# Attention with two MLP layers on one core: batch 0's probabilities turned by TensorE, and a new spread of the MLP's half steps

## The reference

```python
# q, k, v: (4 batches, 8 heads, 576, 64)
scores = scale * q @ k.T
thresh = max(scores, -1) - tau
scores = where(scores >= thresh, scores, -1e9)
attn = exp(scores - max); attn = attn / (sum(attn) + 1e-9)
x = (attn @ v) laid out as 2304 tokens x 512
# layer 0: 512 -> 2048 -> 512
h = x @ w_in;  x = (s * relu(h)**2 + b) @ w_out
# layer 1: 512 -> 2048 -> 512
h = x @ w_in2; out = (h * sigmoid(1.702 * h)) @ w_out2
```

## Time and profile before

| what | value |
|---|---|
| time, median of 3 runs | 1167.25 us (1165.93 to 1169.19) |
| profiled execution | 1167.29 us, its span 1165.5 us |
| PE busy | 1043.8 us (90%) |
| DVE, ACT, POOL busy | 652.5, 650.4, 732.7 us |
| PE busy tenths in 40 slices | 3655678988889988988899999999999999999998 |
| granted TensorE clock over the span | 0.969 of full speed |
| chain that ended last | PE 67%, DVE 15%, POOL 6%, DMA 4% |

### The profile page before, as it was taken

One profiled execution on the slowest core, in us unless ns is written; L12 is line 12 of the kernel. 1 busy time (PEld: TensorE's weight loads), 2 busy tenths in 40 slices (PEclk: granted clock), 3 DMA queues, 4 the chain that ended last, 5 costly groups with the idle time before them and its releaser, 6 DMA issues.

```text
span 1165.5 us, 18156 instructions
## 1 busy us (share of the span) xinstructions
PE 1043.8 (90%) x6024; PEld 915.4 (79%) x6024; DVE 652.5 (56%) x1598; ACT 650.4 (56%) x1215; POOL 732.7 (63%) x773
## 2 busy tenths in 40 slices
PE   3655678988889988998899999999999999999998
PEld 2444467867778877877799999999999998989897
DVE  6988998888889888988223223232222222222222
ACT  3344345665666666666467676654545445454543
POOL 4566556766868777776366566656666666666663
PEclk9976789999999999999999999999999999999999
DMA  3566676787787877766543333433434444444442
GB/s 111 135 160 162 143 180 164 166 187 178 174 199 173 191 184 179 194 168 171 134 127 118 120 125 127 127 121 123 151 125 149 129 126 153 127 154 127 154 127 81
DMA packets 119451, 173.23 MB, mean 149 GB/s; under 512 B 30912, under 2 KB 86336, under 8 KB 119360
## 3 DMA queue, kind: packets, MB, share of 16 engines
q1 hardware_dynamic: 119360, 172.08, 54.7%
HBM read 124.85 MB, written 4.72 MB: 111 GB/s over the span
## 4 chain that ended last, share of the span: by engine, by line
PE 67%; DVE 15%; POOL 6%; DMA 4%; SPq 3%; ACT 2%; issue 2%; DVEq 0%; ACTq 0%; POOLq 0%
PE y_ps L356 28%; PE scores L341 25%; PE shared L341 6%; PE scores L307 5%; DVE scores L413 5%; DVE prob L437 4%; DVE blocks L450 3%; PE scores L286 3%; SPq L225 3%; POOL w_lo L679 3%; DMA prob_t<-blocks 3%; POOL prob L672 1%; POOL q_hl L653 1%; DVE limit L420 1%; DMA qk_raw<-qk 1%
## 5 line engine op out<-in xcount | busy, mean ns | idle before, releaser
L679 POOL TENSOR_TENSOR w_lo<-raw_slab,w_hi 128x512 fp32r<-128x512 f32 x384 | 498.1, 1299 | 291.5 <-ACT w_hi L556 291.0
L473 DVE TENSOR_TENSOR g_lo<-gate,g_hi 128x384 fp32r<-128x384 f32 x192 | 117.8, 614 | 223.9 <-ACT g_hi L584 223.9
L556 ACT CAST w_hi<-raw_slab 128x512 fp32r<-128x512 f32 x384 | 236.0, 616 | 6.1 <-DMA raw_slab<-slabs_a 4.2
L356 PE MATMUL y_ps<-w_lo,g_hi 128*128 128x512 f32 x576 | 227.2, 394 | 0.0
L356 PE MATMUL y_ps<-w_hi,g_lo 128*128 128x512 f32 x576 | 226.8, 394 | 0.0
L356 PE MATMUL y_ps<-w_hi,g_hi 128*128 128x512 f32 x576 | 224.6, 390 | 0.0
L535 ACT ACTIVATE prob<-scores,neg_max 128x576 f32<-128x576 f32 (+1 forms) x160 | 118.5, 740 | 184.3 <-DVE scores L413 181.5
L467 DVE TENSOR_TENSOR gate<-scores,gate 128x384 f32<-128x384 f32 x136 | 75.8, 557 | 194.8 <-ACT gate L566 140.3
L341 PE MATMUL scores<-act_hi,w_hi 128*128 128x384 f32 x544 | 184.7, 340 | 0.0
L341 PE MATMUL scores<-act_hi,w_lo 128*128 128x384 f32 x544 | 183.5, 337 | 0.0
L341 PE MATMUL scores<-act_lo,w_hi 128*128 128x384 f32 x544 | 182.6, 336 | 0.0
(11 more groups left out here) (47 smaller groups left out, 1471.5 us busy)
## 6 DMA issues: line engine op xcount, KB each, us to landing
raw_slab<-slabs_a SPq DMA_DIRECT2D x96, 512.0 KB, 4.2
raw_slab<-slabs_b SPq DMA_DIRECT2D x96, 512.0 KB, 3.5
prob_t<-blocks SPq DMA_DIRECT2D x192, 100.0 KB, 4.1
qk_raw<-qk SPq DMA_DIRECT2D x32, 576.0 KB, 5.4
prob_t<-blocks SPq DMA_DIRECT2D x192, 80.0 KB, 3.7
v_sb<-v SPq DMA_DIRECT2D x16, 320.0 KB, 3.2
out<-rows_b SPq DMA_DIRECT2D x18, 256.0 KB, 4.0
prob_t<-blocks SPq DMA_DIRECT2D x64, 60.0 KB, 2.9
```

The costliest lines, as they stand in the source:

```text
L356: mm = nc.tensor.matmul(y_ps[g][:], gp[:, n % 2, toks], wp[n % W_RING][:, w], start=(f == 0 and k == 0), stop=(f == SLABS - 1 and k == 2))
L473: nc.vector.tensor_tensor(g_lo[:, n % 2, :], gate[:, n % 2, :], g_hi[:, n % 2, :].bitcast(F32), ALU.subtract).then_inc(g_lo_ready, 1)
L556: nc.scalar.copy(w_hi[n % W_RING][:, cols], raw_slab[:, n % 2, cols]).then_inc(w_hi_ready, 1)
L679: nc.gpsimd.tensor_tensor(w_lo[n % W_RING][:, cols], raw_slab[:, n % 2, cols], w_hi[n % W_RING][:, cols].bitcast(F32), ALU.subtract).then_ ...
```

## The change

- Batch 0 (heads 0 to 7) is cut into tiles of 128, 128, 128, 128, 64 rows; the other batches as before (rows_of, cut_of). Its q columns are no longer reordered.
- For these 40 tiles TensorE turns the normalised probabilities, three slots behind their scores: four transposes into y_ps[0] or y_ps[1], a fifth (the last 64 keys) into y_ps[2], for a head's fifth tile into "shared". These banks belong to the MLP, which starts later. ACT copies them into prob_t, or, for pairs 0 and 2, into the idle blocks buffers. DVE's turn and the DMA moves are left for batches 1 to 3.
- Batch 0's contexts are three pieces of 192 columns a pair, at slots 10 x pair + 14, + 16, + 18. Contexts of the other batches come at + 17 to + 20; their moves keep their slots.
- Half steps: 32 over the slots 48 to 91 (8 in 11 slots), from slot 92 on six in five slots; 127 are done at slot 170. The first four slabs are split one part a slot in slots 38 to 45.
- ACT's affine and g_hi come in the slot after the hidden product, g_lo on DVE one later; the turned rows' x_hi and x_lo stand ahead of the gate steps.

```diff
-MLP_FROM = 51
-SECOND_FROM = 91
+MLP_FROM = 48
+SECOND_FROM = 92
+PIECES = [(pair, THIRD * n, THIRD, 2 * TPH * pair + 14 + 2 * n)
+          for pair in range(PAIRS_PER_BATCH) for n in range(3)]
+PIECES += [(pair, RUN * a, QUAD_RUNS[a], 2 * TPH * pair + 17 + a)
+           for pair in range(PAIRS_PER_BATCH, PAIRS) for a in range(QUADS)]
 def halves_by(slot):
+    if slot < SECOND_FROM:
+        return max(0, (2 * SLABS * (slot - MLP_FROM + 1)) // (SECOND_FROM - MLP_FROM))
+    full, rest = divmod(slot - SECOND_FROM, 5)
+    return 2 * SLABS + 6 * full + [1, 3, 4, 5, 6][rest]
+            def turn_tile(j):            # TensorE, in slot j + 3, behind the scores
+                h, t = divmod(j, TPH)
+                m = rows_of(j)
+                if j == 0:
+                    pe.wait_ge(ident_loaded, 16)
+                pe.wait_ge(normed, j + 1)
+                if j >= 2:
+                    pe.wait_ge(main_copied, j - 1)
+                for c in range(KEY_CHUNKS - 1):
+                    nc.tensor.transpose(y_ps[j % 2][:, c * m:(c + 1) * m], prob[0:m, j % PROBS, c * P:(c + 1) * P],
+                                        ident[0:m, 0:m])
+                if t < TPH - 1:
+                    if t == 0 and h >= 1:
+                        pe.wait_ge(tail_copied, h)
+                    place = y_ps[2][0:64, t * P:t * P + m]
+                else:
+                    if h >= 1:
+                        pe.wait_ge(last_copied, h)
+                    place = shared[0:64, 0:m]
+                nc.tensor.transpose(place, prob[0:m, j % PROBS, (KEY_CHUNKS - 1) * P:SEQ], ident[0:m, 0:m]
+                                    ).then_inc(rows_pe_turned, 1)
+            def copy_turned(j):          # ACT, in slot j + 3
+                h, t = divmod(j, TPH)
+                m, q0 = rows_of(j), cut_of(j)
+                act_eng.wait_ge(rows_pe_turned, j + 1)
+                if t == 0 and h >= 4:
+                    act_eng.wait_ge(context_ready, pieces_of(h // 2 - 1))
+                nc.scalar.copy(prob_t_of(h)[:, 0:KEY_CHUNKS - 1, q0:q0 + m],
+                               y_ps[j % 2][:, 0:(KEY_CHUNKS - 1) * m].rearrange("p (c q) -> p c q", q=m)
+                               ).then_inc(main_copied, 1)
...
             # DVE
-            for slot in range(SLOTS):
+            for slot in range(SLOTS + 2):
                 if 0 <= slot - 1 < TILES:
                     mask(slot - 1)
+                if slot - 1 in PIECE_OF:
+                    context_lo(slot - 1)
                 for u in halves_of(slot - 1):
-                    mlp(u)
+                    rows_due(u)
+                for n in hidden_in(slot - 1):
+                    gated(n)
+                for n in hidden_in(slot - 2):
+                    gated_lo(n)
...
             # ACT
+            for slot in range(SLOTS + 1):
                 h, t = divmod(slot, TPH)
+                for n in hidden_in(slot - 1):
+                    affine(n)
                 if slot < TILES:
                     exponent(slot)
+                if slot in PIECE_OF:
+                    context_hi(slot)
+                if 0 <= slot - TURN_LAG < PE_TILES:
+                    copy_turned(slot - TURN_LAG)
+                for n in hidden_in(slot - 1):
+                    gated_hi(n)
                 for u in halves_of(slot):
+                    rows_due(u)
+                for n in hidden_in(slot):
+                    gate_of(n)
+                for u in halves_of(slot):
+                    rows_and_weights(u)
```

More of the change, by code:

```diff
@@ L25 @@
 BLOCKS = SEQ // BLK
-ROWS = [128, 128, 128, 96, 96]
-TPH = len(ROWS)
-CUTS = [sum(ROWS[:t]) for t in range(TPH)]
+ROWS_PE = [128, 128, 128, 128, 64]
+ROWS_DVE = [128, 128, 128, 96, 96]
+TPH = len(ROWS_DVE)
 RUN = TPH * BLK
@@ L186, in build, with prob_t_of @@
         out_written = sem("out_written")
+        def prob_t_of(h):
+            if h < PE_HEADS and h // 2 % 2 == 0:
+                return blocks[h % 2][:].rearrange("p b t j -> p (b t j)").rearrange("p (c q) -> p c q", q=SEQ)
+            return prob_t[h % 2]
         pure_from = halves_by(SLOTS - 1)
@@ L505, in _ @@
                     invert(slot - 2)
-                if 0 <= slot - 3 < TILES:
-                    turn(slot - 3)
-            for u in range(halves_by(SLOTS - 2), HALVES):
-                mlp(u)
+                if PE_TILES <= slot - TURN_LAG < TILES:
+                    turn(slot - TURN_LAG)
+            for u in range(pure_from, HALVES):
+                n = u // 2
+                if n < STEPS and 2 * n >= pure_from:
+                    if u % 2 == 0:
+                        gated(n)
+                    else:
+                        gated_lo(n)
+                rows_due(u)
         @block.scalar
@@ L637, in _ @@
                     split_k(h + 1)
-                if slot in W_EARLY:
-                    for part in range(2):
-                        slab_hi(W_EARLY.index(slot), part)
+                if W_EARLY <= slot < W_EARLY + 2 * W_RING:
+                    slab_hi(*divmod(slot - W_EARLY, 2))
             for u in range(pure_from, HALVES):
-                if u % 2 == 1 and u // 2 < STEPS:
-                    affine(u // 2)
-                mlp(u)
+                n = u // 2
+                if n < STEPS and 2 * n >= pure_from:
+                    if u % 2 == 0:
+                        gate_of(n)
+                    else:
+                        affine(n)
+                        gated_hi(n)
+                rows_due(u)
+                rows_and_weights(u)
         @block.gpsimd
@@ L699, in _ @@
                     split_k(h + 1)
-                if slot in W_EARLY:
-                    for part in range(2):
-                        slab_lo(W_EARLY.index(slot), part)
+                if W_EARLY <= slot < W_EARLY + 2 * W_RING:
+                    slab_lo(*divmod(slot - W_EARLY, 2))
                 for u in halves_of(slot):
```

212 lines of the change are left out of this document (116 added, 96 removed).

## The result

| | before | after |
|---|---|---|
| median, us | 1167.5 (11 runs) | 1171.63 (11 runs, 1168.77 to 1175.65) |
| ratio after / before | | 1.0035, 95% interval 1.002 to 1.0049 |
| span of the profiled execution, us | 1165.5 | 1170.2 |
| forecast, us | | 1148 (range 1137 to 1167) |

A forecast was written before the change was run, and what follows sets the result against it. A 2.50 us round of row_max, exp and mask bounds slots 0 to 50, TensorE the end after the slots; -7.1 - 3.4 - 8.9 = -19.4 on the 1165.5 us span, plus 1.8, gives 1148 us, range 1137 to 1167.

The forecast's parts named there:

- A plain slot stays 2.50: Batch 0 slots: a round of row_max, exp, mask sets 2.50 us, so removing 40 DVE transposes gains 0.
- behind scores(slot) and ahead of scores(slot+1): Batch 0's 200 transposes in TensorE's queue: next scores stay over 0.5 us early, cost 0; +20 if cover goes.
- The clock is up when a pair's first context comes: Batch 0: transposes fill TensorE's slots, so first contexts run at full clock; only one cold context, 1.6 us, counted.
- A: Stage from row_max of slot 0 to that of slot 50, 142.1 us before; forecast 135.0, a change of -7.1.
- Rival 1: Clock stays low in batch 0: four first contexts each pay 1.6 us, +4.9 in all, 1153 us; chance 0.15.
- 12 x 0.5: Batch 0's twelve context pieces of 192 columns, each lengthening its slot by 0.5 us over a plain 2.50.
- B, -3.4: Slots 50 to 92, 142.8 us before: -2.4 fewer halves, -5.0 DMA waits, +4.0 ACT wait.
- +4.0: Slots 50 to 92: ACT's g_hi waits for an output two slots on, four times; +5.1, taken as +4.
- C and D, -8.9: From slot 92 to the end: 2.1 later half, -5 DMA waits, -4 idle filled, -2 paired slots and turns.
- 12.4 forecast: From slot 92: TensorE's act_lo wait at paired slots, 4 x 2.5 + 8 x 0.3, against 14.6 before.
- -4: From slot 92: denser halves shrink TensorE's 5.6 + 3.0 us of waiting for DVE; bounds 0 and -8.6.
- 4 x 2.5: From slot 92: four turns where a hidden step directly follows an output, each waiting 2.5 us for act_lo.

The follow-up runs named there:

- turns_behind_context: Changed kernel, but batch 0's transposes and ACT copies that stood just ahead of a context come behind its scores; 1164.22 us, ratio 0.9950 to the kernel before.
- fill_transposes: Changed kernel plus eight transposes of the identity behind scores in slots 0 to 47 with t 0 to 2, no context; 1165.66 us, 0.9980 of the kernel before.
- fill_matmuls: Changed kernel plus four unused 512-column matmuls behind scores in slots 0 to 47 with t 0 to 2, no context; 1159.19 us, 0.9935 of the kernel before.
- schedule_odd_even: schedule_alone, but in slots 51 to 91 each odd half step comes in the slot right behind its even one; 1153.48 us, 0.9872 of the kernel before.
- schedule_alone: Kernel before, batch 0 still on DVE and DMA, with the new half-step spread, contexts at + 17 and later g_hi, g_lo; 1154.96 us, ratio 0.9883.
- schedule_steady: schedule_alone with one half step a slot from slot 92 on instead of six in five; 1161.42 us, ratio 0.9947 to the kernel before.
- before_filled: Kernel before plus four unused 512-column matmuls in slots 0 to 50 with t below 4 and no context; 1166.90 us, ratio 0.9987.

## Why the prediction was wrong, step by step

- **"A plain slot stays 2.50", the transposes buy nothing.** Right: 2.48 to 2.51 in most of batch 0's plain slots.
- **The transposes on TensorE, priced at 0 from "behind scores(slot) and ahead of scores(slot+1)".** This step failed. The bound was set against the next scores alone. In nine slots the next thing in the queue is a context, which with its scores fills the slot by itself. In six of them the rows come in time and the context starts 0.17 to 0.19 us after row_max all the same. In the other three, the first contexts of slots 14, 24 and 34, the rows come 3.0 us into their slot instead of the 2.0 of the earlier trace rows, because a head's k split stands ahead of them on GpSimd; the context starts 1.7 us late, and this goes straight into the round: 5.1 us in all. Taking the transposes away gave 7.6 us (turns_behind_context), 5.1 in the first contexts' slots and 2.8 in those of the contexts 18 and 38, which then ran at the high clock. The 2.0 us of the earlier trace rows were not laid against the context slots, nor against GpSimd's splits.
- **"The clock is up when a pair's first context comes".** Failed. The clock did rise long before the first context, but it was down again when that came. The averages, 0.84 in A against the 0.81 of the earlier trace rows, mislead: in the kernel before the granted clock reads 1.00 from 10 to 50 us, though the scores matmuls there have the durations of the low level (0.79 to 0.85 us, in the changed kernel 0.53 at the high one). From 50 us on it is 0.74 before and 0.83 after, so the transposes did raise it, too little. The timeline of slots 11 and 12 shows the two scores matmuls at 0.53 us, a wait of 1.78 for GpSimd, and then 0.85:

```profile
38.14 0.53 PE L331 MATMUL scores<-k_hi,q_hl 128*128 128x288 f32 x2
...
40.72 0.68 PE L353 MATMUL y_ps<-ident,prob 64*128 64x64 f32 x4 [1.78 <-POOL prob L782]
...
41.44 0.85 PE L331 MATMUL scores<-k_hi,q_hl 128*128 128x288 f32 x2
```

Rival 1 named this and sized it well for the first contexts: it counted four times 1.6 us, and the four took 6.0 us more than at the high clock. But four later contexts (slots 18, 38, 46, 48) were cold too, 3.47, 2.47, 3.37 and 3.12 us instead of 1.85, another 5.0 that stood in no step. A rule by which transposes do not count for the clock is not the reason, as fill_transposes shows. When exactly the clock falls stays open: in fill_matmuls the same wait of 1.6 us stands ahead of the contexts of slots 24 and 34, and one ran at 3.47, the other at 1.85.
- **"12 x 0.5" for contexts.** Mis-sized: standing alone, a context makes its own slot 2.78 and the next one 3.01, so 0.8 rather than 0.5, 3.5 us in all. With the late start and the low clock gone A is 136.2 us, near the forecast 135.0; the new cut and ACT's copies are in it, so they cost little, as forecast.
- **B, -3.4.** Measured -0.1. The DMA waits of TensorE went as forecast, 6.6 us to none in B and 6.6 to 0.3 in C. The step had priced only that side of the later context: DVE's turn now waits for free blocks (2.5 us in B, 10.7 in C, neither of them before), and TensorE's waits for masks ahead of scores grew from 3.9 to 13.0 in B. Which of these ate the 3.4 us was not tested. The wait on ACT came as forecast, 8.1 us in four waits (about 10 said); schedule_odd_even shows that it cost little, so the +4.0 priced for it was too much.
- **C and D, -8.9.** Measured -6.8, in part by luck. The waits from 306 to 596 us of the changed kernel:

```profile
PE shared L416 <- DVE act_lo L559: 13.1, 7, 3.3
...
DVE blocks L530 <- DMA prob_t<-blocks: 10.7, 12, 1.9
...
PE shared L416 <- POOL w_lo L789: 5.0, 6, 1.3
...
ACT w_hi L658 <- DMA raw_slab<-slabs_a: 4.6, 6, 1.2
```

TensorE waits for act_lo 13.1 us against 12.4 forecast. Its waits for masks and context splits, 5.6 + 3.0 before, are gone whole, where -4 was taken, and the waits for w_lo are new. The four paired turns wait 3.15, 3.32, 1.39 and 2.89 us, 10.8 against 4 x 2.5. In the timeline of slot 98 a part of it is DVE's wait for free blocks, which stands ahead of the mask and x_lo; and the hidden product behind drops to the low clock in the middle (0.33 to 0.52 us a matmul):

```profile
330.58 0.78 DVE L530 STREAM_TRANSPOSE blocks<-prob 128x576 f32<-128x576 f32 x1 [1.95 <-DMA prob_t<-blocks]
...
332.22 0.54 DVE L559 TENSOR_TENSOR act_lo<-shared,act_hi 128x384 fp32r<-128x384 f32 x1
...
332.91 0.41 PE L416 MATMUL shared<-act_hi,w_hi 128*128 128x384 f32 x1 [3.15 <-DVE act_lo L559]
333.16 0.33 PE L416 MATMUL shared<-act_lo,w_hi 128*128 128x384 f32 x1
...
334.39 0.52 PE L416 MATMUL shared<-act_lo,w_hi 128*128 128x384 f32 x1
334.71 0.52 PE L416 MATMUL shared<-act_hi,w_lo 128*128 128x384 f32 x1
```

- **The wait of the hidden product for w_lo** stood in no step. It is new, 5.0 us in C (7.8 in schedule_alone, 2.2 in schedule_steady); the weight loads of the same product had waited 4.3 us for it in C before, and wait 10.1 now. The denser halves overtake GpSimd. One of the prediction's own signs of being wrong came with it: casts waited for raw_slab, 4.6 us in six waits, where the kernel before had one of 0.4.

## What to carry to other kernels

When work is put into an in-order queue, price it against every item that can follow it, and by when its own inputs come. Here it was free in front of 0.8 us of scores and in front of six contexts for which the rows came in time, and cost 1.7 us in front of each of three contexts for which GpSimd was late. A matmul burst behind a half idle stretch can pay in clock as well as in waiting: here 11 us in A, of which a few unused matmuls or transposes in the gaps gave most back, and all only once the late start was gone too. When two repairs together give the sum of each alone, look at the slots before calling them separate. Split a change of many parts by stage and time the parts alone, and then check that they add up: here one half alone won 1.2%, the other alone lost 0.4%, and together they lost 0.35%.

## What the runs showed of the hardware

Four matmuls of 512 columns or eight transposes in three slots of five (none where a context stands) raised the granted clock from 50 to 154 us from 0.83 to 0.97, and shortened stage A by 10.0 and 10.3 us, though TensorE had more to do. Three of the four first contexts were still slow in either (2.87, 3.47 and 3.11 us with the matmuls, 2.65, 3.30 and 3.23 with the transposes, where the high clock gives 1.85). The granted clock of the profile reads 1.00 in the first 40 us of stage A of the kernel before, where the scores matmuls have the durations of the low level (0.85 and 0.68 us a pair, against 0.53 and 0.42): there the durations tell the level. One trace is a weak measure of the later stages: with the same program from slot 51 on, the kernel before took 870.7 us from slot 92 to the end and before_filled 865.8.
